# An attention-and-two-MLP kernel: first transfers and turns reordered at its start, last tiles and last product reordered and split at its end

## What is computed

```python
scores = (q @ k.T) / sqrt(64)
scores = cap * tanh(scores / cap)
attn = exp(scores - max) / (sum + 1e-9)
x = (attn @ v)                       # heads side by side: 896 x 768
h = x @ w_in;  x = (max(h, 0) ** 2) @ w_out     # 768 -> 2048 -> 768
h = x @ w_in2; out = (h * sigmoid(h)) @ w_out2  # 768 -> 2048 -> 768
```

## Time and profile before

| | us |
|---|---|
| median of 3 runs | 545.42 |
| lowest, highest | 544.98, 545.61 |
| the profiled execution's own time | 545.42 |
| span of its trace, first to last instruction | 543.6 |
| busy: PE, DVE, ACT, POOL | 535.0, 375.9, 261.0, 82.2 |

### The profile page before, as it was taken

One profiled execution on the slowest core, in us unless ns is written; L12 is line 12 of the kernel. 1 busy time (PEld: TensorE's weight loads), 2 busy tenths in 40 slices (PEclk: granted clock), 3 DMA queues, 4 the chain that ended last, 5 costly groups with the idle time before them and its releaser, 6 DMA issues.

```text
span 543.6 us, 7023 instructions
## 1 busy us (share of the span) xinstructions
PE 535.0 (98%) x2620; PEld 441.9 (81%) x2620; DVE 375.9 (69%) x597; ACT 261.0 (48%) x403; POOL 82.2 (15%) x54
## 2 busy tenths in 40 slices
PE   7999999999999999999999999999999999999996
PEld 5333334799999999999998999999999999999995
DVE  3299999886778643677789845556855345568985
ACT  4998997064445332444435344454433144454230
POOL 1899999200000000000000000000000000000000
PEclk9999999999999999999999999999999999999999
DMA  7797530151202201412021024202211241020646
GB/s 206 208 230 179 158 98 28 31 137 58 77 2 78 58 1 58 136 58 58 21 77 51 9 59 136 60 21 58 56 50 30 59 134 36 25 78 6 123 66 88
DMA packets 82117, 42.17 MB, mean 78 GB/s; under 512 B 26784, under 2 KB 79008, under 8 KB 82080
## 3 DMA queue, kind: packets, MB, share of 16 engines
q1 hardware_dynamic: 77952, 40.32, 28.5%
q10 hardware_dynamic: 4096, 1.38, 1.1%
q0 software_dynamic: 32, 0.00, 0.0%
HBM read 38.93 MB, written 2.75 MB: 77 GB/s over the span
## 4 chain that ended last, share of the span: by engine, by line
PE 90%; DVE 3%; ACT 2%; DMA 1%; issue 1%; ACTq 0%; DVEq 0%
PE banks L502 26%; PE banks L503 26%; PE banks L504 26%; PE banks L444 6%; PE banks L433 4%; PE banks L452 2%; PE banks L430 2%; DVE w_hl L881 1%; ACT prob L616 1%; DMA qk_raw<-in_q_dram 1%; DVE y L961 1%; ACT prob L622 1%; DMA qk_raw<-in_k_dram 1%; ACT g_hi L699 0%; ACTq L597 0%
## 5 line engine op out<-in xcount | busy, mean ns | idle before, releaser
L502 PE MATMUL banks<-x_hi,w_hl 128*128 128x448 f32 x384 | 140.7, 366 | 0.0
L503 PE MATMUL banks<-x_lo,w_hl 128*128 128x448 f32 x384 | 140.5, 366 | 0.0
L504 PE MATMUL banks<-x_hi,w_hl 128*128 128x448 f32 x384 | 140.5, 366 | 0.0
L502 PE MATMUL banks<-g_hi,w_hl 128*128 128x448 f32 x336 | 123.2, 367 | 0.2 <-DVE w_hl L881 0.2
L504 PE MATMUL banks<-g_hi,w_hl 128*128 128x448 f32 x336 | 122.9, 366 | 0.0
L503 PE MATMUL banks<-g_lo,w_hl 128*128 128x448 f32 x336 | 122.9, 366 | 0.0
L502 PEld LDWEIGHTS banks<-x_hi,w_hl 128*128 128x128 f32 x384 | 72.1, 188 | 7.6 <-issue 1.4
L504 PEld LDWEIGHTS banks<-x_hi,w_hl 128*128 128x128 f32 x384 | 72.1, 188 | 6.2
L503 PEld LDWEIGHTS banks<-x_lo,w_hl 128*128 128x128 f32 x384 | 72.1, 188 | 6.2
L876 DVE TENSOR_TENSOR w_hl<-w_raw,w_hl 128x768 fp32r<-128x768 f32 x32 | 31.4, 981 | 57.4 <-ACT w_hl L648 57.3
L680 ACT ACTIVATE work<-banks 128x448 f32<-128x448 f32 x64 | 31.3, 541 | 77.4 <-PE banks L504 68.4
(11 more groups left out here) (64 smaller groups left out, 550.2 us busy)
## 6 DMA issues: line engine op xcount, KB each, us to landing
w_raw<-in_moe_w_in_dram SPq DMA_DIRECT2D x32, 384.0 KB, 3.4
w_raw<-in_moe_w_out_dram SPq DMA_DIRECT2D x24, 512.0 KB, 5.2
qk_raw<-in_k_dram SPq DMA_DIRECT2D x44, 112.0 KB, 2.6
qk_raw<-in_q_dram SPq DMA_DIRECT2D x44, 112.0 KB, 2.7
v_t<-in_v_dram SPq DMA_DIRECT2D x24, 96.0 KB, 2.7
out_dram<-rows SPq DMA_DIRECT2D x40, 56.0 KB, 2.2
qk_raw<-in_k_dram ACTq DMA_DIRECT2D x4, 112.0 KB, 3.3
qk_raw<-in_q_dram ACTq DMA_DIRECT2D x4, 112.0 KB, 4.2
```

The lines of the kernel that those rows point to most:

```text
L502: pe.matmul(dst, hi[:, kk, :], mov_hi, start=start, stop=False, skip_group_check=onto)
L503: pe.matmul(dst, hi[:, kk, :], mov_lo, start=False, stop=False, skip_group_check=onto)
L504: return pe.matmul(dst, lo[:, kk, :], mov_hi, start=False, stop=stop, skip_group_check=onto)
```

## The change

At the start:

- The first k transfer of SP and of ACT has a semaphore of its own, `s_first_part[0]` and `[1]`. Each of the two engines starts the transfers of pair 1 when its own first one has landed, and no longer waits for all four.
- DVE turns k of pair 0 before it waits for `cap`.
- ACT runs one exp on a zeroed column behind its first four transfers, with the table load before it.
- `WARM` is 11 in place of 14.

At the end, in the last group of the last stage:

- DVE turns tile 0 and tile 1 sooner, and adds to tile 3 later.
- Product n = 6 is made in two column parts, of 256 and of 192 columns, in two banks. Each part is 12 passes with 12 weight loads. Each is subtracted, turned and stored by itself: the last tile goes out in eight transfers of 256 or 192 pieces, not in four of 448.

The diff, cut to its core:

```diff
-    WARM = 14
+    WARM = 11
@@ sync
-            load_head(0, 0, k_v, 0, s_first_in[0])
+            sp.dma_start(qk_raw[0][0:BL, BL:BL + QB * D], k_v[0, 0]).then_inc(s_first_part[0], DMA)
+            sp.dma_start(qk_raw[0][BL:D, 0:QB * D], k_v[0, 0]).then_inc(s_first_in[0], DMA)
             load_head(0, 1, q_v, 0, s_first_in[1])
-            sp.wait_ge(s_first_in[0], 4 * DMA)
+            sp.wait_ge(s_first_part[0], DMA)
             load_head(1, 0, k_v, 0, s_qk_in[1])
...
-                for n in range(4):
+                for n in range(3 if g == GROUPS - 1 else 4):
...
+            for part, t in enumerate(LAST_T):
+                sp.wait_ge(s_rows, 4 * GROUPS + part)
+                for a in range(2):
+                    store(*y_tile(GROUPS - 1, 3), a, t)
@@ tensor, model
+                if layer == 1 and s == 1 and g == GROUPS - 1 and n == NP - 1:
+                    for part, cols in enumerate(LAST_COLS):
+                        for kk in range(KQ):
+                            last = passes(last_bank(part)[:, cols], prod_split(g, n), kk,
+                                          g_hi[:, q, kk, cols], g_lo[:, q, kk, cols], kk == 0, kk == KQ - 1)
+                        last.then_inc(s_prod, 1)
+                    return
@@ scalar
-            act.wait_ge(s_first_in[0], 4 * DMA)
+            act.wait_ge(s_const, 1)
+            act.activation(first_exp[:, :], warm_t[:, 0:1], ACT.Exp)
+            act.wait_ge(s_first_part[1], DMA)
             load_head(1, 0, k_v, 1, s_qk_in[1])
@@ vector
             dve.memset(eps_t[:, :], EPS).then_inc(s_eps_t, 1)
+            for part in range(2):
+                dve.wait_ge(s_first_part[part], DMA)
+            dve.wait_ge(s_first_in[0], 2 * DMA)
+            turn_main(At(0, 0)).then_inc(s_turned, 1)
             dve.wait_ge(s_cap, DMA)
...
-            dve.wait_ge(s_first_in[0], 4 * DMA)
-            turn_main(At(0, 0)).then_inc(s_turned, 1)
             dve.wait_ge(s_first_in[1], 4 * DMA)
...
                         post_u3(layer, s, g)
+                        if last and layer == 1 and s == 1:
+                            post_22(layer, s, g)
+                            turn_rows(g, 0, 5)
+                            prod_low(layer, s, g, 6)
+                            post_11(layer, g)
+                            turn_rows(g, 1, 6)
+                            post_21_u3(layer, g)
+                            post_12(layer, s, g)
+                            break
...
-            post_21(1, 1, GROUPS - 1)
-            leave(1, 1, GROUPS - 1, 3)
+            m, b = y_tile(GROUPS - 1, 3)
+            posted(1, 1, GROUPS - 1, 7)
+            for part, cols in enumerate(LAST_COLS):
+                dve.wait_ge(s_prod, NP * GROUPS * 2 * STAGES + part)
+                add(y[:, m, b, cols], y[:, m, b, cols], last_bank(part)[:, cols],
+                    ALU.subtract).then_inc(s_post, 1)
+                posted(1, 1, GROUPS - 1, 9 + part)
+                dve.transpose(rows[m][:, b, cols], y[:, m, b, cols]).then_inc(s_rows, 1)
```

More of the change, by code:

```diff
@@ L78, in attention_then_two_mlps @@
         eps_t = sb(ctx, "eps_t", [P, 1])
+        first_exp = sb(ctx, "first_exp", [P, 1])
         ones = sb(ctx, "ones", [P, D])
@@ L139, in attention_then_two_mlps @@
         s_first_in = [sem(f"s_first_in{i}") for i in range(2)]
+        s_first_part = [sem(f"s_first_part{i}") for i in range(2)]
         s_turned = sem("s_turned")
@@ L276, in y_bank, with last_bank @@
             return banks[:, (4 if g % 2 == 0 else 0) + i, 0:S]
+        LAST_T = (slice(0, 8), slice(8, QB))
+        LAST_COLS = (slice(0, 8 * BL), slice(8 * BL, S))
+        def last_bank(part):
+            return y_bank(GROUPS - 1, BANK_OF[6]) if part == 0 else y_bank(GROUPS - 2, BANK_OF[0])
         def y_tile(g, n):
@@ L773, in _, with store @@
                             x_high(g, 1)
-            def store(m, b, a):
+            def store(m, b, a, t=slice(0, QB)):
                 cols = slice(m * P + BL * a, m * P + BL * a + BL)
-                act.dma_start(out_v[b, :, :, cols],
-                              rows[m][BL * a:BL * a + BL, b, :].rearrange("p (t r) -> p t r", r=BL)
+                act.dma_start(out_v[b, :, t, cols],
+                              rows[m][BL * a:BL * a + BL, b, :].rearrange("p (t r) -> p t r", r=BL)[:, t, :]
                               ).then_inc(s_out, DMA)
-            for n in range(4):
+            for n in range(3):
                 act.wait_ge(s_rows, 4 * (GROUPS - 1) + n + 1)
@@ L784, in _, with blocks, turn_main, turn_rest @@
                     store(*y_tile(GROUPS - 1, n), a)
+            for part, t in enumerate(LAST_T):
+                act.wait_ge(s_rows, 4 * GROUPS + part)
+                for a in range(2, C):
+                    store(*y_tile(GROUPS - 1, 3), a, t)
         @block.vector
         def _(dve):
+            def blocks(j, first, last):
+                return qk_raw[j.par][:, BL + first * D:BL + last * D].rearrange("p (t x) -> p t x", x=D)[:, :, 0:BL]
+            def turn_main(j):
+                return dve.transpose(qk_f[j.par][:, 0:MAIN].rearrange("p (c g i) -> p g c i", c=CW, g=C),
+                                     blocks(j, 0, MB).rearrange("p (g c) i -> p g c i", c=CW))
+            def turn_rest(j, first, last):
+                return dve.transpose(qk_f[j.par][:, first * BL:last * BL].rearrange("p (t i) -> p t i", i=BL),
+                                     blocks(j, first, last))
             for h in range(2):
@@ L1148, in _ @@
                             w_s3(layer, s, g + 1)
-                        if last and layer == 1 and s == 1:
-                            leave(layer, s, g, 1)
                         if g == 1:
```

25 lines of the change are left out of this document (9 added, 16 removed).

## The result

The changed kernel takes 546.69 us (median of 22 runs, 545.51 to 547.99) against 545.43 us for the kernel before (22 runs on the same chips, 544.88 to 548.21). The ratio is 1.002, with a 95% interval of 1.0013 to 1.0028: slower by 0.13 to 0.28%, where 544.4 was predicted and 545.4 was the upper end of the range. The profiled execution took 546.95 us with a span of 545.2, so it stands 0.26 above its median; the two profiled executions differ by 546.95 - 545.42 = 1.53 us.

What follows compares the result with a forecast made beforehand. PE's products were taken to bound the kernel (PE busy in 98% of the span), leaving only lead and tail to gain: 545.42 - 0.40 - 0.60 = 544.4 us, range 543.7 to 545.4.

Steps and rivals of the forecast that it cites:

- The middle: PE's unbroken products between lead and tail, a stretch of 509 us: number and inputs untouched, so no change in time.
- The lead: Start up to 29.51 us: fewer warm products let scores and first tanh come earlier, gaining 0.40 us, ends 0 to 0.55.
- Rival 2: At the start, pair 1's transfers make q 0.5 us or more late; lead gains nothing, 544.8 us; chance 0.13.
- The delay of q: At the start, pair 1's earlier transfers slow ACT's second q transfer: 0.15 us taken, half of 0.3.
- the cap of 0.36: At the start, PE's slack against ACT limits the lead's gain to 0.36 us if pair 1 lands no sooner.
- Rival 5: At the start, fewer warm products leave first scores at the slow pace: lead -0.8, 545.6 us; chance 0.05.
- The tail: End, after the middle: last product in two parts, last store landed at 542.7 in place of 543.3, gaining 0.6 us.
- rival 4: In the last product, each short pass takes its weight load's whole 0.19 us: 545.9 us, slower; chance 0.07.
- The stores: At the end, ACT's queue, full without a pause before, frees sooner; last store starts at 540.3, lands 2.4 us later.

Runs made afterwards that it cites:

- e1: The kernel before with one unused column (allocated as 32 bytes) where the changed kernel has `first_exp`: 546.47 us, ratio 1.0022.
- e2: The changed kernel with `first_exp` at the end of the attention tiles, where it moves no other tile: 545.03 us, ratio 0.9991.
- e8: The changed kernel with `first_exp` after the attention tiles, 64 unused bytes behind `eps_t`, and pair 1 issued only after all four k transfers: 541.32 us, ratio 0.9917.
- e3: The kernel before with `WARM = 11` and nothing else changed: 545.17 us, ratio 0.9995.
- e9: e8 with a second unused tile of 64 bytes directly behind `w_hl`: 537.23 us, ratio 0.9844.
- e18: e9 with `WARM = 14` in place of 11: 537.2 us, ratio 0.9843.
- e15: e13 with the tail part of the change alone: 537.09 us, ratio 0.9851.
- e14: The changed kernel as given, with 32 unused bytes behind `eps_t` and 64 behind `w_hl`: 537.9 us, ratio 0.986, in two groups of runs.
- e13: The kernel before with 64 unused bytes behind `eps_t` and 64 behind `w_hl`, nothing else changed: 537.92 us, ratio 0.9867.
- e4: The kernel before with an unused tile of 64 bytes at the place of `first_exp`: 542.09 us, ratio 0.9929.
- e17: e14 with `WARM = 14` in place of 11: 537.29 us, ratio 0.9852.
- e16: e13 with the lead part of the change alone, pair 1 issued early: 538.07 us, ratio 0.9877.

## Why the prediction was wrong

- **The middle: the step that failed.** "The change touches neither the number nor the inputs of the products in this stretch of 509 us" is true of the instructions, and I concluded that the stretch stays as long. It became 2.16 us longer. The change did touch a property of the inputs that neither the order nor the trace names, the address: `first_exp`, which I did not weigh at all, moved the weights by 32 bytes against x. e1 gives the loss without the change (1.0022), e2 gives the change without the loss (0.9991). None of my rivals had this in it, and the range was made of the ends alone.
- **The lead: 0.40 forecast, 0.01 measured between the two traces**, and nothing between the middle ones of the two groups above (29.51 and 29.50). Rival 2 came true and not the forecast. The order of the reasoning was right: WARM first, then q, table and turn of k hidden. Two terms were mis-sized. The delay of q, for which I took 0.15 by halving a row of 0.3, is 0.45 in the profiled run and 0.6 in the mean. And the scores were to start 0.05 after the turn of q (7.26 and 7.31); where q is the last thing that they wait for, it is 0.15 (7.72 and 7.87 here, 7.09 and 7.24 in e8, 7.18 and 7.33 in e3). 0.55 - 0.45 - 0.10 leaves nothing. e8 shows the start with pair 1 late: tanh 0.64 earlier than in the kernel before and 0.3 of it at PE's stream, near the cap of 0.36 that I named for pair 1 coming no sooner. But e9 and e18, with the same start, begin their streams at 29.27 and 29.41 and are not faster than e15, which has the old one, so a gain from it is not shown.
- **Rival 5, the slow pace,** had 0.05. A slow clock at the scores is real in part of the runs (e14, and at another place e3), but it came another way than rival 5 has it: in e14 it followed 2.07 us without work, in which PE waited for q, and not a stretch of warm products that was too short. It cost 4.22 - 2.53 = 1.7 us in that trace, more than the 0.8 I gave it, since PE is slow for twelve scores and not only for the first.
- **The tail: 0.6 forecast, 0.6 measured, and that close by luck** (0.83 between the medians of e15 and e13, 0.77 between their traces: 7.03 against 7.80). Passes 0.12 and 0.11 apart as worked out; rival 4, a load in each short pass at 0.19, did not come. Additions and turns of 0.42, 0.45, 0.35 and 0.38 against 0.43, 0.46, 0.36 and 0.39 forecast. The stores are where two errors cancel. The last one was to start 4.51 after the last product's start (540.3 - 535.79) and land 2.4 later. It started 4.78 after it, because the first issue of part 0 took 0.63 us and not 0.5, and the others stand 0.5 apart with 0.47 each; and it landed after 2.0. Nor was the queue what made the tail long. I read ACT's merged row of eight stores as one without a pause. The single rows of the kernel before, the sixth and the seventh store, show one:

```profile
L777 ACTq DMA_DIRECT2D out_dram<-rows x1: 756/756/756, 538.4 to 538.4; - x1
...
L777 ACTq DMA_DIRECT2D out_dram<-rows x1: 581/581/581, 539.8 to 539.8; - x1
```

The sixth is issued by 539.2, the seventh waits for the turned tile of 539.72. The last store began no sooner than in the kernel before, 4.78 us against 4.57 after the last product's start. What the split gained is its landing, 2.0 us for 192 pieces in place of 2.9 for 448.
- **The total.** -0.01 in the lead, +2.16 in the middle, -0.62 in the tail: +1.53, the difference of the two profiled executions. Between the medians it is 1.26; flips that differ from one execution to the next can account for that, but only one execution of each was traced.
- **What was drawn on.** The Trainium skill (Trainium Kernel Development and Optimization, Key Constraints) says that transfers of several queues interleave, and the traces agree: the 0.6 us above is what it came to here. For the middle, the Trainium skill (SBUF — State Buffer, section SBUF: two separate sides) says that only the port pair shared by VectorE and GpSimd causes contention and that "PE, ACT, and DVE's dedicated pair never wait on anyone". That is about engines waiting for each other; whoever takes it to mean that PE's own two operands can lie anywhere is wrong by this case: 200.0 against 203.9 ns a pass in the hidden stages of e4 and of the kernel before, with nothing changed but 64 unused bytes that move the weights against the moving tile.

## The version that beats both

Both kernels are beaten by the kernel before with 64 unused bytes ahead of `ones` and 64 behind `w_hl` (537.92 us), and this by the tail part on top of it (e15, 537.09 us, 0.9851 of the kernel before). e9 (537.23) and e18 (537.20) add the lead with pair 1 issued late, e17 (537.29) adds it with the early issue and 14 warm products; these four can't be told apart. The early issue of pair 1 is best left out: it gains nothing, and e14's two slow runs have it.

## What to carry to other kernels

A new small tile ahead of large ones is not free until its addresses are compared: keep the compiled addresses of stationary and moving tiles the same across a change, or put the new tile behind them, before a difference of a few tenths of a per cent is read as the effect of anything else. Where PE's products fill the time, look at the distance of pass starts by stage; if it varies between stages of equal shape at a full clock, try unused tiles of 32 to 128 bytes between the operands. Where a transfer is on the critical path, try what it gains to start nothing behind it until it has landed. And split a merged row into its single instructions before calling a queue busy without a pause.

## What the runs showed of the hardware that I had not expected

- A pass of 448 columns with a weight load in 32-bit parts costs 200.0, 202.2, 203.9, 204.4 or 205.3 ns by the distance of its two operands modulo 256 bytes; at three distances it stays for tens of us on one of two paces (200.0 or 202.7 against 206.7 ns) and then changes. The granted clock is 1.00 in all of them.
- Much of the spread of the runs goes with it: 544.88 to 548.21 us where stages flip, 537.06 to 537.31 (e9) where none does. Not all: at the same distance e14 and e16, with the early issue, spread over 1.7 us.
- Transfers started 1.0 to 1.5 us sooner (SP at 3.23, ACT at 3.66, against 4.70 and 4.71) made one that was already under way 0.6 us slower in the mean.
